# q and k laid out head dimension first, and the first head prepared alone

## The reference, cut to what matters

```python
def _attn_ref(q, k, v, proj):                       # q, k, v: 2 x 8 heads x 768 x 64
    q_bits = (np.einsum('bhsd,dk->bhsk', q, proj) > 0)   # 6 bits for each query
    k_bits = (np.einsum('bhsd,dk->bhsk', k, proj) > 0)
    q_bucket = np.sum(q_bits * powers, axis=-1)          # powers = 2 ** arange(6)
    k_bucket = np.sum(k_bits * powers, axis=-1)
    mask = q_bucket[:, :, :, None] == k_bucket[:, :, None, :]
    scores = scale * np.matmul(q, k.transpose(0, 1, 3, 2))
    scores = np.where(mask, scores, -1000000000.0)
    scores = scores - np.max(scores, axis=-1, keepdims=True)
    attn = np.exp(scores)
    attn = attn / (np.sum(attn, axis=-1, keepdims=True) + 1e-09)
    return np.matmul(attn, v)
```

## Time and profile before

| | |
|---|---|
| profiled execution: time, span | 846.47 us, 844.7 us |
| median of three runs | 845.37 us |
| PE busy in the span | 789.6 us (93%) |
| DVE busy | 487.7 us (58%) |
| ACT busy | 384.7 us (46%) |
| POOL busy | 312.3 us (37%) |
| attention | from the start to some 297 us |

### The profile page before, as it was taken

One profiled execution on the slowest core, in us unless ns is written; L12 is line 12 of the kernel. 1 busy time (PEld: TensorE's weight loads), 2 busy tenths in 40 slices (PEclk: granted clock), 3 DMA queues, 4 the chain that ended last, 5 costly groups with the idle time before them and its releaser, 6 DMA issues.

```text
span 844.7 us, 14792 instructions
## 1 busy us (share of the span) xinstructions
PE 789.6 (93%) x4442; PEld 708.2 (84%) x4442; DVE 487.7 (58%) x984; ACT 384.7 (46%) x710; POOL 312.3 (37%) x313
## 2 busy tenths in 40 slices
PE   3699999999999799999999999999949999999995
PEld 3599989989988599999999998888837887778784
DVE  5499989989999562222222243455575465555641
ACT  2388888888888541111111123533333355533431
POOL 5266666666777794323432200112100110101110
PEclk9899999999999999999999999999969999999999
DMA  5456756854120032211120021012445355556310
GB/s 171 121 150 158 208 150 132 206 145 98 31 61 1 1 85 78 71 42 37 39 72 0 0 99 64 25 45 106 129 139 194 130 198 173 193 183 240 132 49 21
DMA packets 50392, 88.26 MB, mean 104 GB/s; under 512 B 5789, under 2 KB 24221, under 8 KB 50336
## 3 DMA queue, kind: packets, MB, share of 16 engines
q1 hardware_dynamic: 45648, 76.78, 31.5%
q10 hardware_dynamic: 2448, 4.47, 2.0%
q0 software_dynamic: 2240, 6.31, 1.9%
HBM read 56.94 MB, written 21.04 MB: 92 GB/s over the span
## 4 chain that ended last, share of the span: by engine, by line
PE 71%; DMA 6%; issue 6%; DVE 6%; POOL 4%; ACT 3%; ACTq 2%; DVEq 0%; SPq 0%; POOLq 0%
PE ps_t L857 12%; PE ps_s L809 12%; PE ps_t L708 6%; PE ps_t L924 6%; PE ps_t L809 6%; DMA out_dram<-rows_out,rows_in 6%; PE ps_s L904 5%; PE ps_p L809 3%; PE ps_o L809 3%; PE ps_o L721 3%; PE ps_o L723 3%; POOL probs L539 3%; PE ps_s L694 3%; PE ps_s L696 2%; PE ps_p L665 2%
## 5 line engine op out<-in xcount | busy, mean ns | idle before, releaser
L539 POOL TENSOR_SCALAR probs<-probs,rden,alone 128x768 f32<-128x768 f32 x96 | 93.9, 991 | 87.9 <-DVE rden L1225 87.9
L1231 DVE TENSOR_TENSOR pT_l<-ps_t,pT_h 128x384 fp32r<-128x384 f32 x192 | 97.6, 549 | 9.7 <-ACT pT_h L990 9.4
L1206 DVE TENSOR_REDUCE negmax<-ps_s 128x1 f32<-128x768 f32 x96 | 91.2, 950 | 19.3 <-PE ps_s L696 18.6
L990 ACT ACTIVATE pT_h<-ps_t 128x384 fp32r<-128x384 f32 x192 | 85.5, 492 | 36.8 <-PE ps_t L708 35.6
L809 PE MATMUL ps_s<-xn,w_h 128*128 128x384 f32 x384 | 98.6, 337 | 0.0
L980 ACT ACTIVATE probs<-ps_s,negmax 128x768 f32<-128x768 f32 x96 | 86.9, 906 | 17.3 <-DVE negmax L1206 16.5
L636 POOL DMA_INDIRECT out_dram<-rows_out,rows_in x16 | 23.1, 1442 | 194.0 <-ACT rows_out L1134 194.0
L1366 DVE TENSOR_TENSOR expert_w<-piece,expert_w 128x2048 f32 (+1 forms) x32 | 72.1, 2288 | 33.7 <-ACT expert_w L1102 28.8
L708 PE MATMUL ps_t<-ident,probs 128*128 128x128 f32 x576 | 84.3, 280 | 4.4 <-DVE pT_l L1231 2.3
L904 PE MATMUL ps_s<-expert_w,rowsT_h 128*128 (+1 forms) x256 | 81.8, 401 | 3.6 <-issue 1.9
L924 PE MATMUL ps_t<-expert_w,hidT_h 128*128 (+1 forms) x256 | 80.9, 397 | 3.8 <-DVE expert_w L1366 2.2
(11 more groups left out here) (219 smaller groups left out, 1721.9 us busy)
## 6 DMA issues: line engine op xcount, KB each, us to landing
piece<-in_moe_w_dram SPq DMA_DIRECT2D x32, 1024.0 KB, 6.4
routed<-filler SPq DMA_DIRECT2D x52, 257.0 KB, 5.2
rows_in<-routed ACTq DMA_DIRECT2D x17, 257.0 KB, 2.7
...
```

The lines of the kernel that those rows point to most:

```text
L539: nc.gpsimd.tensor_scalar(pr, pr, rden[:, j:j + 1], alone[:, j:j + 1], ALU.mult, ALU.add).then_inc(norm_done, 1)
L1206: nc.vector.tensor_reduce(negmax[:, c], third(ps_s[j % 2]), AX.XY, ALU.max, negate=True).then_inc(max_done, 1)
L1231: nc.vector.tensor_tensor(pT_l[u % 4][:], ps_t[kt % 2][:, 0:G], pT_h[u % 4][:].bitcast(F32), ALU.subtract).then_inc(low_ready, 1)
```

## The change

The host hands over q and k with the 64 dimensions first (`_dims_first`), so that a head lies on 64 partitions as the products need it. Each is loaded twice, into partitions 0 to 63 and 64 to 127 (`load_qk`, four transfers a pair in place of two, 1.5 MB in place of 0.77). The turns of q and k on PE and the evacuations on ACT are gone. In their place ACT makes rounded copies of 128x768 in four steps of a pair (`high_qk`, `HIGH_STEPS`), and POOL eight differences of 64x384 (`low_qk`). The `lane_scale` column lets one copy give one half of the partitions scaled and one not. SP copies one half of the queries' high part in two transfers instead of the three of before. The projections stand in steps 6, 7, 9, 10 of a pair instead of 3, 4, 8, 9, in pair 0 in 7, 8, 10, 11.

POOL's order within a group is other than before: it now does the differences for the next pair ahead of the group's normalization, and it makes the column `alone` itself (`put_alone`), which was DVE's. The sums of squares for the RMS norm move with it, and the first split of the SwiGLU weights (`split_w(0, 0)`) goes from the middle of pair 7 to its end.

Head 0 of the first pair is loaded and prepared by itself: its bits are written by DVE right where the product reads them, without `bits_m` and a transfer. Head 1 follows in the steps 1 to 4 of pair 0, in the same way.

The diff, cut to its core:

```diff
-TURN_STEPS = (0, 1, 2, 5, 6, 7)
-PROJ_STEPS = (3, 4, 8, 9)
+HIGH_STEPS = (0, 2, 4, 6)
+PROJ_STEPS = (6, 7, 9, 10)
+FIRST_HIGH_STEPS = (5, 6, 7, 8)
+FIRST_PROJ_STEPS = (7, 8, 10, 11)
...
             def load_qk(pair, par):
-                sp.dma_start(rawqk[par][:, KEYS], k_v[:, pair]).then_inc(qk_in[par], 16)
-                sp.dma_start(rawqk[par][:, QUERIES], q_v[:, pair]).then_inc(qk_in[par], 16)
+                for w, src in ((KEYS, k_v), (QUERIES, q_v)):
+                    for half in range(2):
+                        sp.dma_start(raw[par][lanes(half), w], src[pair]).then_inc(qk_in[par], 16)
...
+            def load_first(r):
+                for w, src in ((KEYS, k_v), (QUERIES, q_v)):
+                    for half in range(2):
+                        sp.dma_start(raw[0][lanes(half), w, r], src[0, :, r]).then_inc(first_in[2 * r + w], 16)
...
-            def move_bits(par, w, more):
+            def move_bits(par, w, rows):
                 for r in range(2):
-                    sp.dma_start(more[D:D + 2 * NB, r].rearrange("p t n -> p (t n)").bitcast(F32),
+                    sp.dma_start(rows[D * (1 - r):D * (1 - r) + 2 * NB, r].bitcast(F32),
                                  bits_m[32 * r:32 * r + 2 * NB, w].bitcast(F32)).then_inc(heads_in[par], 16)
...
+            def arrange(R, par):
+
+                for r in range(2):
+                    wait(sp, qk_high, 4 * R + 3 + r)
+                    sp.dma_start(q_a[par][lanes(r), r].bitcast(F32),
+                                 q_b[par][lanes(r), r].bitcast(F32)).then_inc(own_moved, 16)
+                wait(sp, bits_ready, bits_done(R) - 2)
+                move_bits(par, KEYS, k_b[par])
+                wait(sp, bits_ready, bits_done(R))
+                move_bits(par, QUERIES, q_b[par])
 
             def period(P, par, qk=True, vv=True, sw=True):
+                if sw:
+                    arrange(P + 1, 1 - par)
                 if qk:
...
+            load_first(0)
...
+            load_first(1)
...
+            def low_qk(w, r, par, cols):
+
+                part = lanes(r if w == KEYS else 1 - r)
+                dst, high = ((k_b, k_a), (q_a, q_b))[w]
+                nc.gpsimd.tensor_tensor(dst[par][part, r, cols], raw[par][part, w, r, cols],
+                                        high[par][part, r, cols].bitcast(F32), ALU.subtract).then_inc(qk_low, 1)
+
+            def lows_qk(R, par):
+                for n, (w, r) in enumerate(((KEYS, 0), (KEYS, 1), (QUERIES, 0), (QUERIES, 1))):
+                    for half in range(2):
+                        wait_apart(qk_high, 4 * R + n + 1)
+                        wait_apart(qk_low, lows_done(R) - 8 + 2 * n + half)
+                        low_qk(w, r, par, slice(half * G, half * G + G))
+                        yield
...
+            def put_alone(P, g):
+                c = slice(3 * g, 3 * g + 3)
+
+                wait_apart(norm_done, 12 * (P - 1) + 3 * g + 3)
+                wait_apart(max_done, 12 * P + 3 * g + 3)
+                nc.gpsimd.tensor_scalar(alone[:, c], negmax[:, c], MASKED, 1.0 / S,
+                                        ALU.is_ge, ALU.mult).then_inc(alone_put, 1)
+                wait_apart(alone_put, 4 * P + g + 1)
...
+            def period(P, slots, lows_by=(3, 6, 8, 8)):
                 for g in range(4):
-
+                    wait_apart(norm_done, 12 * P + 3 * g)
+                    for n, (steps, count) in enumerate(slots[g]):
+                        if n == 1 and lows_by[g]:
+                            wait_apart(qk_low, lows_done(P) + lows_by[g])
+                        some(count, steps)
+                    if lows_by[g]:
+                        wait_apart(qk_low, lows_done(P) + lows_by[g])
+                    put_alone(P, g)
                     wait_apart(rden_ready, 4 * P + g + 1)
                     for j in range(3 * g, 3 * g + 3):
                         pr = probs[:, j]
                         nc.gpsimd.tensor_scalar(pr, pr, rden[:, j:j + 1], alone[:, j:j + 1],
                                                 ALU.mult, ALU.add).then_inc(norm_done, 1)
-                    for j in range(3 * g, 3 * g + 3):
...
+            def usual_slots(P, par):
+                works_qk, works_v = lows_qk(P + 1, 1 - par), split_v(P + 1, 1 - par)
+                return [(works_qk, 3)], [(works_qk, 3)], [(works_qk, 2), (works_v, 1)], [(works_v, 3)]
...
+            period(0, ([], [(next_qk, 4)], [(next_qk, 4)], [(next_v, 4)]), (0, 4, 8, 8))
...
+            squares = add_squares()
+            period(6, [slot + [(squares, 1)] for slot in usual_slots(6, 0)])
...
+            period(7, ([(squares, 4)], [(squares, 4)], [(squares, 5)], [(squares, 3)]), (0, 0, 0, 0))
+            split_w(0, 0)
...
+            def bits_of(R, par, m, heads, bank):
+
+                w, half = divmod(m, 2)
+                cols = slice(half * G, half * G + G)
+                whole, part = ((k_a, k_b), (q_b, q_a))[w]
+                for n, r in enumerate(heads):
+                    nc.tensor.matmul(bank[:, 0:G], proj_w[:, r, w, 0, :], whole[par][:, r, cols],
+                                     start=(n == 0), stop=False)
+                    mm = nc.tensor.matmul(bank[:, 0:G], proj_w[:, r, w, 1, :], part[par][:, r, cols],
+                                          start=False, stop=(n == len(heads) - 1))
+                mm.then_inc(proj_made, 1)
+
+            def project_bits(R, par, m):
+
+                wait(pe, qk_low, lows_done(R) - 4 + 4 * (m // 2))
+                wait(pe, bits_ready, bits_done(R) - 4 + m)
+                if m == 2:
+                    wait(pe, own_moved, 32 * R)
+                bits_of(R, par, m, range(2), ps_p)
...
+            def project_first(r, m):
+
+                if r == 0:
+                    pe.wait_ge(first_low, 1 + m // 2)
...
+                    pe.wait_ge(qk_low, 2 + 2 * (m // 2))
+                    pe.wait_ge(bits_ready, m + 1)
+                if m == 2:
+                    pe.wait_ge(q_own, r + 1)
+                bits_of(0, 0, m, (r,), first_proj_banks[m])
 
...
+                if isinstance(P, int) and P == 0:
+                    if t == 0:
+                        pe.wait_ge(q_own, r + 1)
+                        pe.wait_ge(bits_ready, 4 * (r + 1))
+                elif j == 0:
+
+                    wait(pe, heads_in[par], heads_until(P, par))
 
                 wait(pe, exp_done, 12 * P + j - 1)
+                queries = slice(t * P128, (t + 1) * P128)
...
+                    if isinstance(P, int) and P == 0 and j in (1, 2, 3, 4):
+                        project_first(1, j - 1)
+                    steps = proj_steps(P)
+                    if ahead and j in steps:
+                        project_bits(P + 1, 1 - par, steps.index(j))
...
+            def high_qk(par, w, r):
+
+                high = (k_a, q_b)[w]
+                at_own = lane_scale[:, (r if w == KEYS else 1 - r):(r if w == KEYS else 1 - r) + 1]
+                nc.scalar.activation(high[par][:, r], raw[par][:, w, r], ACT.Copy, scale=at_own).then_inc(qk_high, 1)
+
+            def own_queries(r):
+                nc.scalar.activation(q_a[0][lanes(r), r], raw[0][lanes(r), QUERIES, r], ACT.Copy,
+                                     scale=SCALE).then_inc(q_own, 1)
+
+            def high_step(R, par, n):
+                if n == 0:
+                    wait(act, qk_in[par], 32 * (R + par))
+                    wait(act, scores_ready, 12 * (R - 1))
+                high_qk(par, n // 2, n % 2)
 
...
-                nc.vector.tensor_scalar(alone[:, c], negmax[:, c], MASKED, 1.0 / S,
-                                        ALU.is_ge, ALU.mult).then_inc(alone_ready, 1)
...
+            def bits_first(r, m):
+
+                w, half = divmod(m, 2)
+                rows, place_ = slice(32 * r, 32 * r + 2 * NB), slice(D * (1 - r), D * (1 - r) + 2 * NB)
+                bits(4 * r + m + 1, bits_ready, (k_b, q_b)[w][0][place_, r, half * G:(half + 1) * G],
+                     first_proj_banks[m][rows, 0:G], w, (k_thr, q_thr)[w][rows, :])
...
+            for w, (low, high) in enumerate(((k_b, k_a), (q_a, q_b))):
+                part = lanes(w)
+                dve.wait_ge(qk_high, w + 1)
+                nc.vector.tensor_tensor(low[0][part, 0], raw[0][part, w, 0], high[0][part, 0].bitcast(F32),
+                                        ALU.subtract).then_inc(first_low, 1)
+            dve.wait_ge(cleared, 2)
             for m in range(4):
-                bits(0, m, first_proj_banks[m])
...
+def _dims_first(a):
+    b, h, s, d = a.shape
+    t = s // P128
+    return a.reshape(b, h // 2, 2, P128, t, d).transpose(0, 1, 5, 2, 4, 3).reshape(b * h // 2, d, 2, s)
```

306 lines of the change are left out of this document (129 added, 177 removed).

## The result

| | before | after |
|---|---|---|
| median | 844.83 us (4 runs) | 864.86 us (4 runs: 864.22 to 866.21) |
| ratio, 95% interval | | 1.0239 (1.0218 to 1.026) |
| profiled execution: time, span | 846.47, 844.7 us | 864.22, 862.4 us |
| first maximum | 29.33 | 14.57 |
| pair 0 (first maximum to the next pair's) | 28.25 | 39.12 |

The forecast was 852 us, in a range of 837 to 864: the side was right, the size was not. The rows of the table add up: -14.8 + 10.9 + 23.3 + 0.1 - 1.8 = +17.7 us, and the profiled executions differ by 17.75.

The account below looks back on a forecast made before the run. PE leads (31.51 of 31.81 us in pair 2) with DVE close behind, so relieving PE alone gives little. -15.0 + 9.6 + 9.6 + 0.9 + 1.2 = +6.3 us on 846.47, forecast 852 us; eight-in-ten range 837 to 864.

Parts of the forecast that it names:

- Start, -15.0: Kernel start: head 0's earlier preparation brings the first maximum 15.0 us earlier, to 14.3 us.
- Pair 0, +9.6: Pair 0: late copies, differences and last bits lengthen it from 28.25 to 37.9 us, +9.6 us.
- End of a pair, 6.8 us with a wait of about 2.3 for the transfer: Pairs 1 to 6, step 10 to next first maximum: 6.8 us in place of 4.8, PE standing about 2.3.
- Pairs 1 to 6, inside, 26.8 us: Pairs 1 to 6, first maximum to that of step 10: 26.8 us against 27.0, nothing gained.
- step 5 is 0.6 us late: Pairs 1 to 6, step 5: group 0's normalization waits behind POOL's third difference and ACT's copy, 0.6 us late.
- At most some of 1.5 us a pair: Pairs 1 to 6: taking 24 transposes a pair off PE gives at most some of 1.5 us a pair.
- near 28 us a pair: Sign to look for in the pairs: PE busy near 28 us a pair.
- Soft waits: Rival for the pairs: PE runs a step ahead, DVE without gaps, pairs of 30.8 us, kernel 830 us; chance 0.24.
- The clock: Rival at pair boundaries: new waits halve PE's clock, about 1.5 us more at each of seven, 863 us; chance 0.19.
- Pair 6's squares, +0.9: Pair 6: squares ahead of its normalization add 0.9 us.
- Pair 7, +1.2: Pair 7 and after: squares ahead of normalizations +0.4, extra sums of squares +0.8; nothing changes from there on.

Follow-up runs that it names:

- e5: Changed kernel with pair 0's copies for pair 1 in steps 2 to 5 (not 5 to 8) and bits in 6, 7, 9, 10: 856.3 us.
- e4: Changed kernel with ACT's second copy of keys at step 1, not 2, and the last two projections and bits one step earlier (steps 8, 9): 850.7 us.
- e1: Changed kernel with ACT's second copy of the next pair's keys one step earlier (step 1 in place of 2): 859.4 us.
- e3: Changed kernel with ten extra unused products on PE ahead of the transfer wait at the start of pairs 1 to 7: 863.9 us.
- e11: Kernel with all orders early and `alone` on DVE (839.5 us), plus 24 transposes a pair put back on PE in pairs 1 to 6: 840.0 us.

## Why the prediction was right in its side and wrong in its size

- **Start, -15.0:** right (-14.8 in the profiled execution; the first maximum stands at 14.4 to 15.8 in the others).
- **Pair 0, +9.6:** right in kind and nearly in size (+10.9). Its turns of groups 1 and 2 stand behind POOL, whose differences wait for ACT; e5 took that away and with it 8.1 us of the pair.
- **End of a pair, 6.8 us with a wait of about 2.3 for the transfer:** right (6.7; 1.9). e4 shows it.
- **Pairs 1 to 6, inside, 26.8 us: this is the step that failed** (28.8), by two terms. The first is the chain into step 5. It was the right one, "step 5 is 0.6 us late", but its size was read from pair 7 of before, which stands outside the hardware loop, as a copy of 0.8, a difference of 1.0 and 0.3 "for `alone` and its waits": 2.1 us. From the end of step 2's exponential sum (134.41) to the normalization it is 3.2 in pair 3: copy 0.93, a wait of 0.33 from ACT to POOL, difference 1.00, then 0.52, 0.24 and 0.30 for `alone` and the waits on its two sides (the copy begins 0.1 ahead of the sum's end). In pair 5, outside the loop, it is 2.3, and step 5 takes 3.2 us, near the 3.1 of the forecast (2.5 and 0.6), where pairs 1 to 4 take 4.8. So most of what this term lacked are POOL's waits inside the loop; why they are longer there no run shows. With a wait of 0.23 there already, the whole excess fell on PE. e1 confirms place and kind.
- **The second term is the clock,** which the sum put at nothing. Six falls at boundaries cost 3.7 us by e3, and two behind step 5 some 1.2 each by its neighbouring pairs: an estimate of 6 of the 12.8 us below.
- **"At most some of 1.5 us a pair" for PE's turns:** right, and rather nothing (e11: 0.3 us in all). PE busy "near 28 us a pair" was wrong: it is 31.4, and 29.9 at full clock. The turns had been counted at 3.7 us a pair from their own rows, which overlap other products; e11's 24 add 1.57 to PE's busy time.
- **The rivals.** Soft waits: refuted. The clock: it fell at six boundaries of seven, as that rival said, and in pairs 2 and 4 behind step 5 as well, but a boundary's fall costs 0.6 us by e3 where 1.5 were priced. That 863 was close to the time is chance: its sum had the wrong terms.
- **Pair 6's squares, +0.9:** right. Pair 6 takes 35.2 us and pair 5, worked by POOL outside the loop like it but without squares, 34.4; the whole difference is in step 5 (3.95 and 3.16), where a square of 0.83 us stands ahead of the normalization. **Pair 7, +1.2:** right inside the pair (+1.0: 28.3 in place of 27.2 us from first to last maximum), but the 22.3 us behind it were 21.4, without the half clock of the earlier trace rows. The rest of the kernel took 1.8 us less in the profiled execution.

By size, against 852.8 for the profiled execution: pairs 1 to 6 +12.8 beyond the forecast, pair 0 +1.3, start +0.2, the rest -2.9; together 864.2.
